# Another order of loads and of all engines in a top-k attention and MLP kernel on one core

## What is computed

```python
batch, n_heads, seq, head_dim = (4, 8, 576, 64)
scores = scale * np.matmul(q, k.transpose(0, 1, 3, 2))            # scale = 1/8
kth = np.partition(scores, -top_k, axis=-1)[..., -top_k:-top_k + 1]  # top_k = 32
scores = np.where(scores >= kth, scores, -1000000000.0)
attn = np.exp(scores - np.max(scores, axis=-1, keepdims=True))
attn = attn / (np.sum(attn, axis=-1, keepdims=True) + 1e-09)
out = np.matmul(attn, v)
x = out.transpose(0, 2, 1, 3).reshape(2304, 512)
h = x @ w_in                                                     # 512 x 2048
g = h * np.tanh(np.where(h > 20.0, h, np.log1p(np.exp(np.minimum(h, 20.0)))))
y = g @ w_out                                                    # 2048 x 512
```

## Time and profile before

| | us |
|---|---|
| median of 3 runs | 767.41 |
| the profiled execution | 767.29 |
| its span | 765.4 |
| DVE busy | 699.7 |
| PE busy | 719.3 |
| ACT busy | 583.7 |
| POOL busy | 541.3 |

### The profile page before, as it was taken

One profiled execution on the slowest core, in us unless ns is written; L12 is line 12 of the kernel. 1 busy time (PEld: TensorE's weight loads), 2 busy tenths in 40 slices (PEclk: granted clock), 3 DMA queues, 4 the chain that ended last, 5 costly groups with the idle time before them and its releaser, 6 DMA issues.

```text
span 765.4 us, 14092 instructions
## 1 busy us (share of the span) xinstructions
PE 719.3 (94%) x4952; PEld 558.1 (73%) x4952; DVE 699.7 (91%) x1512; ACT 583.7 (76%) x975; POOL 541.3 (71%) x698
## 2 busy tenths in 40 slices
PE   4658899999999999999999999999999999999998
PEld 2235677777787878777877777777787878777886
DVE  6798999999999999999999999999999999999400
ACT  4878878787878787878787878788787878787831
POOL 1775677676868686858586868686868686777743
PEclk9868999999999999999999999999999999999999
DMA  7631000012122000010110000012122000000000
GB/s 250 210 110 36 11 5 8 21 39 87 43 90 76 23 8 21 24 53 23 56 42 22 8 21 9 21 39 87 42 89 78 18 11 18 12 15 1 15 1 27
DMA packets 23397, 33.93 MB, mean 44 GB/s; under 512 B 2592, under 2 KB 11808, under 8 KB 23328
## 3 DMA queue, kind: packets, MB, share of 16 engines
q1 hardware_dynamic: 21456, 29.63, 11.9%
q10 hardware_dynamic: 1872, 3.41, 1.4%
HBM read 28.31 MB, written 4.72 MB: 43 GB/s over the span
## 4 chain that ended last, share of the span: by engine, by line
DVE 71%; PE 11%; issue 9%; ACT 3%; POOL 2%; DMA 2%; SPq 0%; ACTq 0%; POOLq 0%
DVE p_sb L749 36%; DVE top L756 28%; DVE top L738 6%; PE ps_y L477 2%; PE ps_s L366 2%; PE ps_u L435 1%; DMA g_tok<-w_in 1%; PE ps_o L413 1%; PE ps_y L481 1%; DMA k_sb<-k_in 1%; PE ps_u L454 1%; PE ps_y L454 1%; POOL p_sb L816 1%; PE ps_s L385 1%; PE ps_u L440 1%
## 5 line engine op out<-in xcount | busy, mean ns | idle before, releaser
L756 DVE MAX8 top<-p_sb 128x8 f32<-128x576 f32 x432 | 307.2, 753 | 0.0
L749 DVE MATCH_REPLACE8 p_sb<-top,p_sb 128x576 f32<-128x576 f32 x288 | 213.0, 749 | 0.0
L816 POOL TENSOR_TENSOR p_sb<-x_sb,p_sb 128x576 f32<-128x576 f32 x144 | 202.5, 1427 | 13.9 <-ACT p_sb L564 13.9
L564 ACT ACTIVATE p_sb<-x_sb,limit 128x576 f32<-128x576 f32 x144 | 107.8, 772 | 65.2 <-POOL limit L806 65.1
L831 POOL TENSOR_SCALAR p_sb<-p_sb,recip 128x576 f32<-128x576 f32 x144 | 106.4, 749 | 67.0 <-DVE recip L719 66.0
L573 ACT ACTIVATE p_sb<-p_sb,neg_max 128x576 f32<-128x576 f32 x144 | 111.1, 772 | 22.8 <-POOL p_sb L816 22.4
L477 PE MATMUL ps_y<-w_hi,g_hi 128*128 128x512 f32 x288 | 119.0, 413 | 0.0
L435 PE MATMUL ps_u<-win_hi,xT_hi 128*128 128x512 f32 x288 | 117.6, 408 | 0.3 <-ACT raw L627 0.2
L477 PE MATMUL ps_y<-w_lo,g_hi 128*128 128x512 f32 x288 | 112.8, 392 | 0.0
L435 PE MATMUL ps_u<-win_lo,xT_hi 128*128 128x512 f32 x288 | 112.7, 391 | 0.0
L738 DVE MAX8 top<-x_sb 128x8 f32<-128x576 f32 x144 | 102.7, 750 | 8.3 <-ACT x_sb L555 8.3
(11 more groups left out here) (57 smaller groups left out, 1025.1 us busy)
## 6 DMA issues: line engine op xcount, KB each, us to landing
v_sb<-v_in SPq DMA_DIRECT2D x32, 320.0 KB, 3.5
k_sb<-k_in SPq DMA_DIRECT2D x16, 288.0 KB, 3.1
q_sb<-q_in SPq DMA_DIRECT2D x69, 64.0 KB, 1.8
y_out<-y_sb SPq DMA_DIRECT2D x16, 256.0 KB, 2.0
g_tok<-w_in SPq DMA_DIRECT2D x4, 512.0 KB, 4.3
pT<-w_in SPq DMA_DIRECT2D x4, 512.0 KB, 5.0
raw<-w_out ACTq DMA_DIRECT2D x8, 256.0 KB, 2.8
y_sb<-w_out ACTq DMA_DIRECT2D x5, 256.0 KB, 2.6
```

What stands on the lines that cost most here:

```text
L564: act.activation(p_sb[:, s % PS_, t, :], x_sb[:, s % XS, t, :], ACT.Relu, bias=limit[:, s % TS, t:t + 1], scale=-BLOW_UP).then_inc(penalty ...
L749: dve.match_replace(out=left[:, t, :], in_to_replace=best[:, t, EIGHT * r:EIGHT * r + EIGHT], in_values=x[t] if r == 0 else left[:, t, :], ...
L756: dve.max(best[:, t, EIGHT * r + EIGHT:EIGHT * r + 2 * EIGHT], left[:, t, :]).then_inc(found, 1)
L816: pool.tensor_tensor(p, x_sb[:, s % XS, t, :], p, ALU.subtract).then_inc(arg_ready, 1)
```

## The change

What it does:
- SP loads k of pair 1 right behind the first queries, and all pieces of w_in and w_out, in one list written out ahead of the loop; ACT issues no load any more. Each load waits in that list for its place to be free.
- The last w_in piece (7) is staged in g_tok instead of pT, so it waits for piece 6, and copy_pT(1) waits for six pieces instead of eight.
- INVERSE_AT is (30, 26, 32, 31) instead of (31, 29, 35, 33).
- PE, ACT and POOL have other orders in their loops.

```diff
-INVERSE_AT = (31, 29, 35, 33)
+INVERSE_AT = (30, 26, 32, 31)
...
+        def in_place(c):
+            return 0 if c == ICHUNKS - 1 else c % 2
...
+            def load_w(c):
+                if c >= WP:
+                    sp.wait_ge(wlow_made, c - WP + 1)
+                sp.dma_start(w_stage(c), w_out[P * c:P * c + P, :]).then_inc(wout_loaded[c % WP], 16)
...
-                    sp.wait_ge(inlo_ready, c - 1)
+                    sp.wait_ge(inlo_ready, c if c == ICHUNKS - 1 else c - 1)
...
-            for c in range(WP):
-                load_w(sp, c)
+            load_k(1)
             load_in(0)
             load_in(1)
-            for g in range(1, PPB):
-                load_k(g)
+            load_w(0)
+            load_k(2)
+            load_k(3)
+            load_w(1)
+            load_w(2)
             for pr in range(PPB):
                 load_v(pr, 0)
...
-                if c + WP < FT:
-                    load_w(act, c + WP)
...
-                    act.wait_ge(inlo_ready, ICHUNKS)
+                    act.wait_ge(inlo_ready, ICHUNKS - 2)
```

More of the change, by code:

```diff
@@ L513, in _ @@
                 up(m, 3)
+                low_w(12 * m + 23)
                 transposes(4 * m + 6)
-                low_w(12 * m + 25)
+                low_w(12 * m + 24)
                 down(m, 0)
-                scores(4 * m + 10)
                 turn(m, 2)
                 turn(m, 3)
+                scores(4 * m + 10)
+                low_w(12 * m + 25)
+                down(m, 1)
                 low_w(12 * m + 26)
[L521 to L524, removed]
         @block.scalar
@@ L639, in _ @@
             for m in range(FIRST_ROUND, BLOCKS + 1):
+                exp(4 * m + 4, 0)
+                split_in(8 * m + 10)
+                exp(4 * m + 4, 1)
                 split_in(8 * m + 11)
-                exp(4 * m + 4, 0)
-                exp(4 * m + 4, 1)
-                copy_low(12 * m + 18)
+                split_w(12 * m + 16)
+                copy_xT(m)
                 copy_x(4 * m + 7, 0)
-                copy_low(12 * m + 19)
                 penalty(4 * m + 5, 0)
                 copy_x(4 * m + 7, 1)
-                copy_xT(m)
@@ L649, in _ @@
                 penalty(4 * m + 5, 1)
-                split_in(8 * m + 12)
[L651 to L655, removed]
+                copy_low(12 * m + 15)
+                copy_g(m - 1, 3)
+                split_w(12 * m + 17)
+                copy_pT(4 * m + 4, 0)
+                copy_pT(4 * m + 4, 1)
+                split_in(8 * m + 12)
                 exp(4 * m + 5, 0)
@@ L657, in _ @@
                 exp(4 * m + 5, 1)
-                split_w(12 * m + 21)
[L659 to L669, removed]
+                copy_x(4 * m + 8, 0)
@@ L670, in _ @@
+                split_w(12 * m + 18)
+                copy_low(12 * m + 16)
+                copy_x(4 * m + 8, 1)
+                mish(m, 0)
+                copy_low(12 * m + 17)
+                copy_low(12 * m + 18)
+                split_in(8 * m + 13)
+                split_w(12 * m + 19)
+                penalty(4 * m + 6, 0)
+                penalty(4 * m + 6, 1)
+                split_w(12 * m + 20)
+                split_in(8 * m + 14)
+                split_w(12 * m + 21)
                 copy_pT(4 * m + 5, 0)
@@ L671, in _ @@
                 copy_pT(4 * m + 5, 1)
-                copy_low(12 * m + 22)
-                split_w(12 * m + 24)
+                copy_low(12 * m + 19)
+                copy_y(m - 1)
+                copy_g(m, 0)
+                split_w(12 * m + 22)
                 exp(4 * m + 6, 0)
+                copy_low(12 * m + 20)
                 exp(4 * m + 6, 1)
-                copy_g(m, 0)
                 copy_g(m, 1)
-                copy_y(m - 1)
-                copy_low(12 * m + 23)
-                split_w(12 * m + 25)
+                copy_low(12 * m + 21)
@@ L691, in _ @@
                 exp(4 * m + 7, 0)
+                split_w(12 * m + 25)
+                split_in(8 * m + 17)
                 exp(4 * m + 7, 1)
+                copy_g(m, 2)
+                split_w(12 * m + 26)
+                copy_x(4 * m + 10, 0)
+                copy_x(4 * m + 10, 1)
+                penalty(4 * m + 8, 0)
+                copy_low(12 * m + 24)
+                penalty(4 * m + 8, 1)
+                split_in(8 * m + 15)
                 copy_low(12 * m + 25)
-                copy_x(4 * m + 10, 0)
-                split_in(8 * m + 17)
                 copy_low(12 * m + 26)
-                copy_x(4 * m + 10, 1)
                 split_w(12 * m + 27)
[L699 to L707, removed]
                 copy_pT(4 * m + 7, 0)
                 copy_pT(4 * m + 7, 1)
-                split_w(12 * m + 30)
-                split_w(12 * m + 31)
         @block.vector
@@ L828, in normalise @@
                 pool.wait_ge(recip_ready, s + 1)
-                for t in range(2):
+                for t in tiles:
                     p = p_sb[:, s % PS_, t, :]
@@ L840, in _ @@
                 negate(4 * m + 5)
+                split_xT(m)
                 normalise(4 * m + 4)
-                split_xT(m)
                 exponent(4 * m + 5, 0)
                 exponent(4 * m + 5, 1)
+                split_in(8 * m + 11)
+                guard(4 * m + 5)
+                normalise(4 * m + 5, (0,))
                 split_in(8 * m + 12)
-                guard(4 * m + 5)
+                normalise(4 * m + 5, (1,))
+                negate(4 * m + 6)
                 split_in(8 * m + 13)
[L848 to L851, removed]
                 split_g(m - 1, 3)
@@ L855, in _ @@
                 split_g(m, 0)
+                negate(4 * m + 7)
                 guard(4 * m + 6)
-                split_in(8 * m + 16)
-                negate(4 * m + 7)
                 normalise(4 * m + 6)
@@ L869, in _ @@
                 split_in(8 * m + 18)
+                split_in(8 * m + 15)
                 split_g(m, 2)
-                split_in(8 * m + 19)
 def kernel(q, k, v, moe_w_in, moe_w_out):
```

76 lines of the change are left out of this document (48 added, 28 removed).

## The result

The change makes the kernel faster by about 4 us: 763.39 us (median of 10 runs, 761.44 to 765.76) against 767.43; the ratio is 0.9943, 95% interval 0.9926 to 0.996. A second set of runs on another chip gave 764.13 against 767.07, ratio 0.9952 (0.9931 to 0.9973). I had forecast 769.1. The time lies near the first rival (762.4), but not for the rival's reason.

A forecast was written before the change was run, and what follows sets the result against it. VectorE (DVE), with 71% of the chain of waits, was taken to bound the kernel. Start -3.6, blocks +6.75 and end -1.4 summed to +1.7 us, on the median 769.1 us; range 761 to 774.

The forecast's parts named there:

- first rival: Blocks: the cycle has 0.5 us to spare, so DVE stays without idle time; 762.4 us, chance 0.33.
- Part 1: Start (loads, weight pieces, orders of the first two rounds): saves 3.6 us of DVE waits, ends 0.7 and 8.1.
- the sum of the new waits: Start: DVE's waits, 9.5 us without the first load, become 5.9 us, between 1.4 and 8.8.
- my best end: Start: waits of 1.4 us if every PE piece runs at full clock and each load takes 4.0 us.
- the largest waits before reciprocals 2 and 3: Start: sign that waits before 90 us total 4 to 8 us, largest before reciprocal 2 or 3.
- The walk: Start: new lists followed in each engine's order, giving times for exps, guards and DVE's waits.
- the late end: Start: with PE slow throughout by the skill's rule, waits sum to 8.8 us, 2.9 us later than forecast.
- Part 2: Every block: DVE waits 0.45 us for the denominator of duo 4m+7, in blocks 1 to 15, 6.75 us in all.
- T: Blocks: the moment DVE ends duo 4m+5; denominator due at T + 31.64 us, wanted at T + 31.17.
- Just enough: Blocks: guard of duo 4m+5 ends at 8.2 us after DVE ends that duo, against its place at 8.3; cost 0.
- Part 3: End: PE's 1.50 us wait before transposes(69) goes; gain 1.4 us, ends 0 and 1.5.
- second rival: Start stays as late as before, PE at half clock, 8 us of waits before 90 us; 772.1 us, chance 0.20.

The follow-up runs named there:

- x3: New loads, orders and reciprocal places only up to block 0, those of before from round 1 on; 760.31 us against 767.69 for the kernel before, ratio 0.9905.
- first profile: Profiled execution of the changed kernel in its first set of runs; 761.98 us against 767.29 for the kernel before.
- x10: The changed kernel with 60 small filler matmuls in PE's gaps of rounds -2 to 0, nothing else; 761.64 us, ratio to before 0.9924.
- x9: New start, orders of before in rounds 1 to 15, new from 16, plus 60 filler matmuls, also before transposes(4); 757.87 us, ratio to before 0.9872.
- x1: The changed kernel with INVERSE_AT (30, 26, 32, 33), so reciprocals of duos 4m+7 stand two places later; 761.18 us, ratio 0.9914.
- second profile: Profiled execution of the same changed kernel, run again on another chip, span 764.1 us; that set's median 764.13 us, ratio to before 0.9952.

## Why the prediction was wrong

- **Part 1, the sum of the new waits: this is the step that failed.** I put 5.9 us for 9.5, with 1.4 and 8.8 as its ends, so the start was to save 3.6 us. By x3 it saves 7.4. The waits measured 0.42 us in the first profile, below my best end; 2.64 and another 1.44 in block 0 in the second; and with PE kept busy 1.29 (x10) and 0.59 (x9). With 7.4 in place of 3.6 my own sum would have come to -2.0 us instead of +1.7. I had the largest waits before reciprocals 2 and 3; neither has one in the two profiles. Reciprocal 0 was right: guard(0) started at 26.81 us and DVE passed at 28.21 without a wait (I had 27.8 and 27.9). The walk held up to guard(1), started at 35.52 for 35.5. From there my times were too late against the first profile: guard(2) at 49.56 for 50.4 to 51.5, guard(3) 57.72 for 59 to 64, guard(4) 66.36 for 68 to 75.
- I find two reasons for that. First, the clock. I chose a middle value because of the 0.67 from 40 to 60 us; that number belonged to the old order, in which PE stood still for 4.9 us before single scores. In the new order its longest wait there is 2.1 us (before 60.51), and the granted clock of the stretch was 1.00 in the first profile and 0.83 in the second, where PE had waited 3.3 us before 38.44. I carried a condition of the old order into the new one. Second, I added up durations where starts follow each other faster: in the start of the changed kernel a 128x512 copy lasts 0.59 to 0.62 us by its record, but the next instruction starts 0.48 to 0.52 us after it. Some ten such records lie between two exps; that would be 1 us for each duo, an estimate. It is worked out from rows, no run took it apart, and how the 3.8 us that I missed (7.4 less 3.6) divide between the two reasons is not shown.
- The Trainium skill (TensorE: Matmul & The Clock Gate, section What's actually happening) gives the half rate after idleness as the rule; by it I had put the sum at the late end. The trace bears out that the clock falls behind gaps, and the fillers moved the median by 2.5 us. But the same gap of 3.1 us led to both rates in two executions, so the rule alone doesn't give the time, and the late end that I worked out by it (8.8 us) is twice what the slower profile shows (4.1).
- **Part 2** was right in its mechanism, place and order of size: 0.36 us a block for 0.45. The terms: T to transposes 4.23 us for 4.32 (negate's pair took 0.46, not 0.57), 21.88 for 21.90 to mish, 5.39 for 5.42 to the denominator. 0.36 in 15 blocks is 5.4 us for 6.75; the table has 5.1. PE's waits for pT turned into 1.15 us before transposes(4m+4), as foretold. "Just enough" for duo 4m+5 was short by 0.14 us as soon as the other wait was gone (x1).
- **Part 3** was right: 1.5 us gained for 1.4.
- So the sum was -9.1 + 0.3 + 5.1 - 1.5 in the first profile where I had -3.6 + 6.75 - 1.4. The second rival (start saves nothing, PE at half clock) named a cause that is there, with the wrong size: the waits of the start and block 0 are 4.1 us in the slower profile, not 8, some 2.1 of them behind the half rate, and its time is still below the time before. The first rival had the time right for the wrong reason: the blocks do wait. That was luck, a start better than it assumed and blocks worse.
- The stated ends of the range were not the walk's own: 767.4 - 8.1 - 1.4 is 757.9 us, not 761, and the worst ends of all parts give 777.2, not 774.

## What to carry to other kernels

An order that is good in the start need not be good in the loop: here the halves had opposite signs (-7.4 and +6 us), so test and write them apart, and look for what the seam between them costs (1.1 us here). Bounds for a PE that idles between pieces have to be made for the gaps of the new order, not taken from the clock of the old one; and add starts, not durations. When executions of one kernel differ by more than usual, look at the granted clock of the start before trusting a median, and try to close the gap ahead of the first long run of matmuls, by order or with harmless matmuls.

## What the hardware showed that I had not expected

With 60 small matmuls that compute nothing the kernel's median fell by 2.5 us (764.13 to 761.64) and its times agree within 1.4 us. Behind the same idle time of 3.1 us PE came back at full rate in one execution and at half rate in another, and a start that differs by this much shows in the end time almost one for one, 700 us later: the second profile has 3.7 us more of waits before 102 us and a span longer by 3.9, because DVE has next to no idle time in between to take it up.
